# Attention and the first layer on one core: the last two batches' attention placed between the first layer's matmuls

## What is computed

```python
# attention: q, k, v are (4, 8, 576, 64); keys and values are averaged over 8 tokens
k_p = k.reshape(B, H, 72, 8, D).mean(axis=3); v_p = v.reshape(B, H, 72, 8, D).mean(axis=3)
scores = (q @ k_p.T) / sqrt(64); attn = softmax(scores)          # rows of 72
x = (attn @ v_p) -> (B * S, H * D) = (2304, 512)
# first layer: w_in (512, 2048), w_out (2048, 512)
h = x @ w_in; g = 0 where h <= -1, h where h >= 1, (h + 1)**2 / 4 between; x = g @ w_out
# second layer, same sizes
h = x @ w_in; g = max(h, 0) + log1p(exp(-|h|)); out = g @ w_out
```

## Time and profile before

| what | us |
|---|---|
| median of 3 runs | 885.12 (884.27 to 890.27) |
| the profiled execution, whole | 888.39 |
| its span, first to last instruction | 885.9 |
| PE busy in the span | 845.2 |
| DVE, ACT, POOL busy | 647.8, 456.5, 419.5 |

### The profile page before, as it was taken

How to read it: one execution, slowest core, us unless ns; L and a number is a source line. 1 busy time by engine, 2 the same in 40 slices (tenths; PEclk the granted TensorE clock), 3 DMA queues, 4 the chain that set the end, 5 groups by cost and what they waited for, 6 DMA issues and landing times.

```text
span 885.9 us, 12883 instructions
## 1 busy us (share of the span) xinstructions
PE 845.2 (95%) x4986; PEld 827.0 (93%) x4986; DVE 647.8 (73%) x671; ACT 456.5 (52%) x668; POOL 419.5 (47%) x297
## 2 busy tenths in 40 slices
PE   6886899999999999999999999999999798999998
PEld 5664799999999999999999999999999798999998
DVE  4999647444445697969767599898899979769642
ACT  3787543222222353534445777887887645344532
POOL 6899326556445444224000298898856606221000
PEclk8999699999999999999999999999999899999999
DMA  8984117657545597553551335666655694755532
GB/s 184 197 195 117 47 54 232 219 172 241 205 170 196 197 361 288 209 220 133 223 190 55 89 125 183 230 207 210 217 186 180 223 399 183 242 209 195 201 122 71
DMA packets 106536, 167.77 MB, mean 189 GB/s; under 512 B 21872, under 2 KB 94448, under 8 KB 101872
## 3 DMA queue, kind: packets, MB, share of 16 engines
q1 hardware_dynamic: 101280, 162.28, 55.3%
q10 hardware_dynamic: 5200, 4.72, 1.6%
HBM read 96.21 MB, written 70.78 MB: 188 GB/s over the span
## 4 chain that ended last, share of the span: by engine, by line
PE 80%; DVE 13%; ACT 4%; issue 1%; DMA 1%; SPq 0%; DVEq 0%; ACTq 0%
PE ps L1081 40%; PE ps L1099 34%; DVE xs L871 4%; DVE t_a L914 2%; PE ps L1025 2%; DVE ops L927 2%; ACT qT L579 1%; PE ps L1052 1%; DVE den L842 1%; PE ps L1114 1%; DMA q_raw<-in_q_dram 1%; DVE Tm L881 1%; DVE t_a L917 1%; PE ps L1011 1%; PE ps L1139 1%
## 5 line engine op out<-in xcount | busy, mean ns | idle before, releaser
L1081 PEld LDWEIGHTS ps<-xs,W 128*128 128x128 f32 x2304 | 400.9, 188 | 2.0 <-issue 2.0
L1081 PE MATMUL ps<-xs,W 128*128 128x384 f32 x2304 | 402.4, 335 | 0.0
L1099 PE MATMUL ps<-xs,Tm 128*128 128x384 f32 x1968 | 347.2, 336 | 9.7 <-DVE xs L871 9.2
L1099 PEld LDWEIGHTS ps<-xs,Tm 128*128 128x128 f32 x1968 | 343.2, 189 | 11.0 <-issue 10.0
L637 ACT ACTIVATE xs<-ops 128x768 fp32r<-128x768 f32 (+1 forms) x148 | 111.7, 825 | 158.2 <-PE ps L1099 146.3
L513 POOL TENSOR_TENSOR ops<-ops 128x384 f32<-128x384 f32 x48 | 65.3, 1361 | 232.2 <-DVE ops L927 128.0
L871 DVE TENSOR_TENSOR xs<-ops,xs 128x768 fp32r<-128x768 f32 (+1 forms) x148 | 168.5, 1198 | 0.0
L656 ACT ACTIVATE t_a<-t_a 128x768 f32<-128x768 f32 x48 | 40.7, 849 | 137.2 <-DVE t_a L896 137.2
L896 DVE TENSOR_SCALAR t_a<-ps 128x768 f32<-128x768 f32 x48 | 45.9, 956 | 79.9 <-PE ps L1081 79.6
L940 DVE TENSOR_TENSOR X<-ps,X 128x768 f32<-128x768 f32 x41 | 38.6, 954 | 73.3 <-PE ps L1099 73.3
L927 DVE TENSOR_TENSOR ops<-t_a,t_b 128x768 f32<-128x768 f32 x48 | 62.0, 1292 | 21.5 <-ACT t_b L676 20.2
(11 more groups left out here) (63 smaller groups left out, 706.3 us busy)
## 6 DMA issues: line engine op xcount, KB each, us to landing
gops<-ops SPq DMA_DIRECT2D x48, 1344.0 KB, 5.8
ops<-gops SPq DMA_DIRECT2D x36, 1536.0 KB, 7.3
X<-gops SPq DMA_DIRECT2D x22, 384.0 KB, 6.3
w_raw<-in_moe_w_in_dram SPq DMA_DIRECT2D x32, 256.0 KB, 3.7
t_raw<-in_moe_w_out_dram SPq DMA_DIRECT2D x6, 1024.0 KB, 10.0
k_raw<-in_k_dram SPq DMA_DIRECT2D x16, 288.0 KB
q_raw<-in_q_dram SPq DMA_DIRECT2D x32, 144.0 KB, 6.2
v_raw<-in_v_dram SPq DMA_DIRECT2D x16, 288.0 KB
```

The source lines that it names most:

```text
L1081: last = mm(banks[:, tb, :], W[:, slot, f, part, c * P:(c + 1) * P], x[:, x_part, at:at + TB], start=c == 0 and s == 0, stop=c == KC - 1 a ...
L1099: last = mm(banks[:, d, :], Tm[:, t, part, j, d * P:(d + 1) * P], g[:, g_part, at * TB:(at + 1) * TB], start=at == 0 and s == 0, stop=at = ...
```

## The change

Units 0 to 7 (batches 0 and 1) are computed ahead, as before but without hardware loops. Units 8 to 15 are spread over the half-quads of tiles 0 and 1, four units per tile. After `make_h(0, a)` for `a` below 32 each engine runs `shared_turn(a)`: a unit takes three turns (r = 0, 1, 2), and what it holds is shown in the diff. While that lasts `make_h` has two bank pairs (banks 2, 3 and 6, 7) and `ops` has two slots, the third slot's memory holding the raw inputs of one unit; from `a` = 32 on it is four and three again. Scores are one matmul per head and block, K = 64 rows of the array each, 20 a unit with 72 columns; `kT` is plain and copied at once. Loads for the shared units are issued by ACT, POOL makes all three pooling sums for them, and the remainders of tiles 1 and 2 of the first layer go from POOL to DVE, at fixed half-quads.

```diff
-BANKS_OF = (1, 3, 2, 0)
+TURNS = 2 * JJ
+SHARED = 2 * TURNS
+SHARED_BANKS, ALL_BANKS = (1, 3), (2, 0, 1, 3)
...
+        def turn_of(t):
+            tile, r = divmod(t, TURNS)
+            a, r = divmod(r, 3)
+            u = FIRST + PAIRS * tile + a
+            return u, r, 1 <= a <= PAIRS, a < PAIRS
...  SP
-            with sp.Fori(1, B - 1) as b:
-                load_batch(b)
+            load_v(4)
             load_weights(0, 0)
+            load_v(5)
             load_weights(0, 1)
+            load_v(6)
+            load_v(7)
+            load_shared(FIRST)
             load_weights(0, 2)
...  POOL
+            def shared_sums(t):
+                u, r, old, new = turn_of(t)
+                if r == 1 and old and u - 1 > FIRST:
+                    pool_values(u - 1)
+                if r == 2 and new and u + 1 < UNITS:
+                    pool_keys(u + 1)
...
+            pool_values(4)
+            pool_values(5)
+            pool_values(6)
             fill_lo_piece(0, 0)
+            lo_w(0, 0)
+            pool_values(7)
             fill_lo_piece(0, 1)
+            pool_keys(FIRST)
             fill_lo_piece(0, 2)
             fill_lo_piece(0, 3)
+            pool_values(FIRST)
...
+                    if layer == 0 and 2 * k < SHARED:
+                        shared_sums(2 * k)
+                        shared_sums(2 * k + 1)
                     s_sums(layer, k)
...  ACT
-                    for h in range(2 if a == 1 else 0):
-                        rows = slice(h * HD, (h + 1) * HD)
-                        last = nc.scalar.activation(kT[rows, h * SP:(h + 1) * SP],
-                                                    ps[rows, 1, K_COL:K_COL + SP], ACT.Copy)
+                    if a == 1:
+                        last = nc.scalar.activation(kT_u[:, :], ps[:, 1, K_COL:K_COL + SP], ACT.Copy)
...
+            def shared_turn(t):
+                u, r, old, new = turn_of(t)
+                if r == 0:
+                    if old:
+                        copy_p(u - 1, 0)
+                    if new:
+                        copy_qk(u)
+                    if old and u - 1 > FIRST:
+                        load_shared_v(u - 1)
+                elif r == 1:
+                    if old:
+                        copy_p(u - 1, 1)
+                    if new:
+                        if u + 1 < UNITS:
+                            load_shared_qk(u + 1)
+                        for h in range(2):
+                            exp_scores(u, h)
+                elif old:
+                    store_x(u - 1)
+                    fill_hi_piece(fill_of(0, t // TURNS + 1), (u - 1) % PAIRS)
...  DVE
+                if r == 1 and new:
+                    for h in range(2):
+                        take_max(u, h)
+                    for h in range(2):
+                        shift(u, h)
+                elif r == 2 and new:
+                    weights_of(u)
...
                             clip(a)
-                            if a > 0:
+                            if a < SHARED:
+                                shared_turn(a)
+                                larger(a)
+                                if a % TURNS >= 6 and a % 3 == a // TURNS and a % TURNS < 6 + 3 * PIECES:
+                                    fill_lo_piece(a // TURNS + 1, (a % TURNS - 6) // 3)
+                            elif a > SHARED:
                                 larger(a - 1)
...  PE
+            def score(u):
...
+                for i in range(NS):
+                    for h in range(2):
+                        rows = slice(h * HD, (h + 1) * HD)
+                        last = mm(ps[0:SROW, (2 if u < FIRST else 4) + h, i * SP:(i + 1) * SP],
+                                  qT_of(u)[rows, i * SSTEP:i * SSTEP + SROW], kT_of(u)[rows, :], start=True, stop=True)
...
+            def shared_turn(t):
+                u, r, old, new = turn_of(t)
+                if r == 0:
+                    if old:
+                        transpose_p(u - 1, 0)
+                    if new and u > FIRST:
+                        transpose_qk(u)
+                elif r == 1:
+                    if old:
+                        transpose_p(u - 1, 1)
+                    if new:
+                        score(u)
+                elif old:
+                    attend(u - 1)
...
+            for i in range(1, FIRST):
+                turn(i)
+            make_h(0, 0, range(0, 1))
+            turn(FIRST)
+            make_h(0, 0, range(1, 3))
+            turn(FIRST + 1)
+            make_h(0, 1, range(0, 3))
+            transpose_qk(FIRST)
+            make_h(0, 0, range(3, KC))
+            make_h(0, 1, range(3, KC))
+            shared_turn(1)
             for layer in range(2):
-                for a in range(1 if layer == 0 else 0, HPAIRS):
+                for a in range(2 if layer == 0 else 0, HPAIRS):
                     make_h(layer, a)
+                    if layer == 0 and a < SHARED:
+                        shared_turn(a)
```

More of the change, by code:

```diff
@@ L38 @@
 UNITS = B * PAIRS
+FIRST = UNITS // 2
+REST = UNITS - FIRST
 QR = 6
@@ L489, in _ @@
             for j in range(PAIRS):
-                pool_keys(0, j)
-            pool_batch(0)
-            with pool.Fori(1, B - 1) as b:
-                pool_batch(b)
+                pool_keys(j)
+            for j in range(PAIRS):
+                pool_values(j)
+                pool_keys(PAIRS + j)
             def fill_lo_piece(n, piece):
@@ L834, in turn @@
+            def turn(i):
+                u, old, new = i, 0 <= i < FIRST, i <= FIRST - 2
                 if old:
+                    rows = prob[:, u % PAIRS, :, :, :].rearrange("p h i s -> p (h i) s")
+                    d = den[:, u % 2, :, :].rearrange("p h i -> p (h i)")
                     dve.wait_ge(exped, 2 * u + 2)
@@ new lines, in transpose_p @@
+            def transpose_p(u, h):
+                pe.wait_ge(prob_ready, u + 1)
+                if u < FIRST:
+                    wait(pe, p_copied, 2 * u)
+                elif h == 1 and u % PAIRS < PAIRS - 1:
+                    for bank in range(2):
+                        pe.wait_ge(qk_copied[bank], u + 2)
+                elif h == 1:
+                    pe.wait_ge(x_stored, u)
+                bank = 4 + 2 * h if u < FIRST else (4, 0)[h]
+                for i in range(NS):
+                    n = SROW if i == NS - 1 else SSTEP
+                    col = i % NS_A * SSTEP
+                    last = nc.tensor.transpose(ps[0:SP, bank + i // NS_A, col:col + n],
+                                               prob_of(u, h)[0:n, i, :], ident[0:n, 0:n])
+                last.then_inc(p_transposed, 1)
@@ L1049, in attend @@
+            def attend(u):
+                pe.wait_ge(p_copied, 2 * u + 2)
+                if u < FIRST:
+                    pe.wait_ge(v_summed, u + 1)
+                    for bank in range(2):
+                        pe.wait_ge(qk_copied[bank], min(u + 5, FIRST))
+                    if u >= FIRST - 4:
+                        pe.wait_ge(x_stored, u)
+                else:
+                    pe.wait_ge(v_pooled, u - FIRST + 1)
                 for half in range(2):
-                    pe.wait_ge(qk_copied[half], copied)
```

495 lines of the change are left out of this document (254 added, 241 removed).

## The result

The changed kernel took **892.9 us** (median of 20 runs, 889.2 to 902.5), the kernel before 888.0 in the same sessions (20 runs, 883.5 to 891.2). The ratio is 1.0076, with a 95% interval of 1.0051 to 1.0102: 5 to 9 us slower, about the 1% that was called "no change", but on the other side of what was forecast. The profiled execution has a span of 892.5 us where before had 885.9, so there are 6.6 us to find.

A forecast was written before the change was run, and what follows sets the result against it. The prediction took a PE-ACT-PE loop to bound the attention stage and PE's unbroken matmuls the first layer. Minus 44, plus 31, minus 2, plus 9 gave minus 6 us: 885.1 to 879, range 865 to 896.

The forecast's parts named there:

- What goes: Attention stage ahead of the first layer: eight units leave, with fewer disturbances and key copies, 44 us less.
- The disturbances before 115 us stay in kind: Front before the first layer: tile 0's pieces still made beside the last units ahead; only 1.5 us less taken.
- What comes: PE work of eight units between the first layer's half-quads: 3.9 us each, 31 us, less 2 us for the new scores.
- Putting small work between large costs nothing by itself: First layer: small PE work between half-quads adds only its own time, read from six transposes between products.
- By the rows a change costs about nothing: Turn from `attend` to `score`: no hole seen, so four changes of tiling mode a unit were given no price.
- What waits: Shared stage, tile ends and start: waits of 5 + 2 + 1 + 1 = 9 us, between 1 and 30.
- The 5 us for loads: Shared stage: PE waits for values and keys whose loads land late behind stores or POOL's sums, over 8 units.
- rival 3: Third turn of each shared unit: `den` waits for POOL's sums, 2 us in 8 units, plus 16, about 893; chance 0.12.
- the stages keep their lengths: Behind the first layer: the change touches nothing there, so no stage changes length.
- loads behind stores: Shared stage: all ACT's loads land behind stores, 30 us in place of 5, plus 19, 904 us; chance 0.12.
- row halves not side by side: Scores of 16 units: 2.45 us each, 20 us more, plus 16 in all, 901 us; chance 0.07.
- nothing waits: Shared stage: loads land between stores and DVE stays ahead, minus 15, 870 us; chance 0.24.

The follow-up runs named there:

- e_warm: Changed kernel with 49 idle 128 by 128 matmuls put into the last attention turns ahead and between the first chunks; 890.7 us, ratio 1.0056 to the kernel before.
- e_best: Changed kernel with the weight split earlier, chunks in order of ready pieces, unit 8's copies and last remainders earlier; 886.4 us, ratio 0.9999 to the kernel before.
- e_chain_free: Changed kernel with half-quads 0 and 1 using chunks 0 and 1 twice, not waiting for tile 0's last two pieces; 888.3 us, ratio 1.0029.
- e_switch: Kernel before with small matmuls (whole array, row halves, column halves) and transposes added ahead of the first layer's half-quads; 925.1 us in one run.
- e_no_load: Changed kernel without the loads of units 9 to 15, which compute on unit 8's data; 891.1 us, ratio 1.0063 to the kernel before.
- e_piece_early: Changed kernel with the last remainders of tiles 1 and 2 made one half-quad earlier; 892.0 us, ratio 1.0058 to the kernel before.
- e_full_shared: e_best with scores of units 8 to 15 on all 128 rows, keys padded with zeros in two copies; 894.8 us, ratio 1.0056 to the kernel before.
- e_grouped: Changed kernel with a unit's scores run head by head instead of alternating between row halves; 909.4 us, ratio 1.0170 to the kernel before.
- e_best_again: Same code as e_best, unchanged, measured again beside other runs of the kernel before; 883.9 us, ratio 0.9977.

## Why the prediction was wrong

**What goes: 44 us forecast, 39.6 measured.** Half-quad 1 was to be done at 76. Two steps failed. First, "The disturbances before 115 us stay in kind". They didn't: the eight turns that went held them too, so that by `attend` two units before the last the front was 49.9 us shorter (55.6 against 105.5), not 44. And POOL's load was taken to be lighter in the new order, since only one L499 and the L506 came together. In truth POOL's queue from 53.3 to 67.4 us was one run of two pieces, a weight, two poolings and a third piece, and PE's last turns and chunks hung on it in series: 10.2 us more than before from `attend` of unit 5 to half-quad 1. Some of this is half clock, since PE's operations there took twice their time; but e_warm needs 22.2 with none, e_best 13.9 with half clock for its first 2.4 us only, and e_chain_free, which frees the last two pieces, 16.7. Second, the clock was carried over as "stays in kind", while the stage ahead lost it: 44 us of half clock before half-quad 1's end after, 27.3 before. By the two traces of e_best's code, 10.2 us less at half clock were worth 6 us there. The record also has the mean granted clock of each execution. Its median is 0.971 over the 20 runs of the changed kernel, about 52 us at half clock, and 0.983 over 123 runs of before, about 30. Over the changed kernel's runs (all but the one of 902.5 us, which shows 0.989) the time grew by 0.19 us for each us at half clock. So some 4 us of the loss may be clock, ahead of the first layer and behind it together; this is an estimate from a correlation, and no run holds the clock and nothing else.

**What comes, PE's work: 3.65 us a unit forecast, 4.35 measured.** From half-quad 1 to 32 that is 34.2 us (eight units less the turning of unit 8's queries, which is done before) in place of 29: 5.2 us. This is the largest single miss, though the sum would have stayed above zero without it. The step that failed is "Putting small work between large costs nothing by itself", with "By the rows a change costs about nothing". Both readings were of rows that couldn't show it. The earlier trace rows has transposes between products, which change no tiling (0.00 to 0.03 us in e_switch). And the 0.18 us between the 1.23 us of the scores and the 1.41 of the chain was put down to "the end of `attend`"; it stands just where `attend` on column halves gives way to scores on the whole array, and e_switch shows 0.155 to 0.21 us for such a change. The rule of the Trainium skill that I weighed at nothing (TensorEngine Tiling (Array Packing), Tiling Modes: a changed mode drains the array) was the right one to price: the runs agree that a change costs time, 0.155 us going in and 0.21 coming back. The score itself, taken as 1.0, measured 1.015 plus 0.155 for entering. `attend`'s entry lies in its own 1.12 us, forecast as 1.1, so that changes of tiling are some 4.6 of the 5.2 us.

**What waits: 9 us forecast.** 43.3 - 34.2 leaves 9.1 us, so the sum came out right, but by luck: 1.6 us of it are clock and no wait, and the places were others. Before `score(8)` PE stood 2.1 us, and half-quad 2 lost some 1.6 to half clock (5.96 us, 4.39 at full clock with the change of tiling); behind it the view of waits has 4.1 us, and 1.3 us are in no view's row. The 5 us for loads were 0.4 (e_no_load: 0.6). Tile ends: 1.3 in the view (2 forecast), 2.2 by e_piece_early. Three waits for scaled weights took 2.4 us in all, which the sum had only as a small share: rival 3 in small. PE's idle time from 80 to 250 us was 5.5 us, within the 5 to 15 of the sign, but not most of it ahead of `attend` and `transpose_qk`, as was said.

**What the change doesn't touch: 0 forecast, 2.9 us measured.** The second layer and the products do the same work, but "the stages keep their lengths" failed. The changed kernel was at half clock for 3.4 us at 367.3 and at 756.4 us, behind idle time of PE that both kernels have. Both stretches in the changed kernel's trace:

```profile
363.70:368.70 5.00, 3.01 (x14) 2.72 (x13) 5.00 (x4) 3.05 (x4) 2.32 (x1) 0.86 0.16 67
...
755.00:765.00 10.00, 9.50 (x46) 9.51 (x47) 7.30 (x9) 1.26 (x2) 0.00 (x0) 0.83 0.68 238
```

The first kind stands in 12 of the 16 traces of the changed kernel and its variants, the second in 10, and neither in the three traces of the kernel before (two) and e_switch. Matmul by matmul against the trace of before, the changed kernel falls behind by 1.45 us in each of the two stretches and by next to nothing elsewhere: together they are the 2.9 us. Whether that is chance or due to where the stages fall in time isn't settled, and no run here could try it.

**The sum again:** -6 forecast; +4.4 for the front, +5.2 for PE's work, +0.1 for waits, +2.9 behind, is +6.6, the difference of the spans. Of the rivals, loads behind stores and row halves not side by side are refuted, `den` waiting for POOL was 2.4 us of 16, and "nothing waits" failed on a term that it shared with the forecast. "I am wrong if half-quad 1 ends later than 80 us" fired at 80.2, and so did the sign on changed lengths behind the first layer. One reading of the page was off: in the first five slices PE is at 6 to 8 tenths, not 5 to 8; nothing hangs on it.

A repaired change is about level with the kernel before: e_best 0.9999 and 0.9977, both intervals reaching over 1.0. The median of 883.9 against 886.9 leaves room for a small gain that these runs can't tell from none.

## What to carry to other kernels

Matmuls on halves of the array placed between whole-array matmuls cost 0.37 us for each excursion, whatever their number, so it should pay to put a unit's half-array work into one excursion (not tried here), or to keep it where PE waits anyway. When work moves away from in front of a stage, write out the queue of every engine up to that stage's first operand: here tile 0's pieces, which before were all there 6 us before PE asked for them, became the path. And read small unexplained remainders in a chain (0.18 us here) as a price with a cause, before multiplying by the number of times the change repeats it.

## What the hardware showed that I had not expected

- Whole array to halves: 0.155 us on entering, 0.21 on going back, for row and column halves alike; transposes between them and whole-array matmuls 0 to 0.03 (e_switch).
- A float32 matmul of 116 by 72 on the whole array takes 0.20 us, nearly as long as one of 144 columns (0.245): halving the columns saved a fifth (e_full_shared).
- Row halves gain only when they alternate: 1.17 against 1.83 us for ten matmuls (e_grouped), and 2.00 on the whole array (e_full_shared).
- Two executions of one program were granted half clock for 34 and for 24 us before half-quad 1, at other places, and it ended 6 us apart (e_best, e_best_again); the changed kernel's runs spread over 13 us, those of before over 8.
- A clock row can be incomplete: e_grouped shows full clock over operations that took twice their usual time.
